# An attention head with a PSUM bank pair per item, and remainders and state additions ahead of the spline in every fourth step

## The reference

```python
f = 1.0 / (1.0 + np.exp(-f_logit))
for t in range(S):
    state = f[:, :, t, :, None] * state + np.einsum('bhd,bhe->bhde', k[:, :, t], v[:, :, t])
    y[:, :, t] = np.einsum('bhd,bhde->bhe', q[:, :, t], state)
# x = y as (3072, 384); layer 1, w_in 384 x 2048, w_out 2048 x 384:
h = x @ w_in
x = np.where(h >= 1, h, np.where(h <= -1, 0, (h + 1) ** 2 / 4)) @ w_out
# layer 2, same shapes:
h = x @ w_in2
P = a[0] + a[1] * h + a[2] * h**2 + a[3] * h**3
Q = 1.0 + abs(b[0]) * abs(h) + abs(b[1]) * h**2
out = (P / (Q + 1e-6)) @ w_out2
```

## Time and profile before

| | us |
|---|---|
| median of 3 runs | 1020.75 |
| lowest, highest | 1018.28, 1024.6 |
| the profiled execution's own time | 1022.0 |
| its span | 1020.3 |

### The profile page before, as it was taken

How to read it: one execution, slowest core, us unless ns; L and a number is a source line. 1 busy time by engine, 2 the same in 40 slices (tenths; PEclk the granted TensorE clock), 3 DMA queues, 4 the chain that set the end, 5 groups by cost and what they waited for, 6 DMA issues and landing times.

```text
span 1020.3 us, 12881 instructions
## 1 busy us (share of the span) xinstructions
PE 938.0 (92%) x4626; PEld 756.8 (74%) x4626; DVE 747.9 (73%) x909; ACT 573.0 (56%) x725; POOL 253.5 (25%) x138
## 2 busy tenths in 40 slices
PE   3589898988999899989989997999999999999996
PEld 3467777777777777777778775788888888888885
DVE  6677775666666666657735669998888888888884
ACT  4434433443433344334324468888878788787872
POOL 4123320000001000000003433523434435243223
PEclk9698889999999999999999998999999999999999
DMA  5333321211121121113012231001001010010000
GB/s 163 96 95 90 92 63 51 74 32 31 51 59 31 31 79 32 45 47 87 1 32 75 80 93 62 1 1 62 0 21 41 0 62 0 0 62 0 31 1 34
DMA packets 27510, 48.68 MB, mean 48 GB/s; under 512 B 5312, under 2 KB 8384, under 8 KB 27456
## 3 DMA queue, kind: packets, MB, share of 16 engines
q1 hardware_dynamic: 27456, 48.00, 15.9%
HBM read 36.18 MB, written 9.44 MB: 45 GB/s over the span
## 4 chain that ended last, share of the span: by engine, by line
PE 72%; DVE 15%; ACT 6%; issue 5%; POOL 1%; POOLq 0%; DMA 0%; SPq 0%; ACTq 0%; DVEq 0%
PE acc L1086 18%; PE h_pair L1026 14%; PE acc L1042 13%; PE at_pair L1064 9%; PE h_pair L1064 9%; DVE t L832 4%; PE at_pair L971 3%; DVE g L839 3%; DVE x_lo L827 2%; ACT t L589 2%; PE at_pair L989 2%; PE at_bank L998 1%; PE at_pair L984 1%; ACT g_hi L596 1%; DVE growth L765 1%
## 5 line engine op out<-in xcount | busy, mean ns | idle before, releaser
L832 DVE SCALAR_TENSOR_TENSOR t<-t 128x512 f32<-128x512 f32 x96 | 85.7, 893 | 127.7 <-ACT t L589 126.8
L487 POOL TENSOR_TENSOR g_lo<-g,g_hi 128x1024 fp32r<-128x1024 f32 x48 | 116.7, 2431 | 233.1 <-DVE t L867 228.6
L589 ACT ACTIVATE t<-h_pair,half 128x512 f32<-128x512 f32 x96 | 65.9, 687 | 162.2 <-PE h_pair L1026 161.2
L596 ACT CAST g_hi<-g 128x512 fp32r<-128x512 f32 x96 | 59.5, 620 | 148.9 <-DVE g L839 148.3
L1026 PE MATMUL h_pair<-x_hi,w_hi 128*128 128x512 f32 x288 | 116.8, 405 | 16.1 <-DVE x_lo L827 15.6
L1042 PE MATMUL acc<-g_hi,w_hi 128*128 128x512 f32 x288 | 119.6, 415 | 0.0
L449 POOL TENSOR_TENSOR k_s<-k_in,growth 128x512 f32<-128x512 f32 x24 | 32.9, 1371 | 342.0 <-DVE growth L765 342.0
L1042 PE MATMUL acc<-g_hi,w_lo 128*128 128x512 f32 x288 | 115.8, 402 | 0.0
L1042 PE MATMUL acc<-g_lo,w_hi 128*128 128x512 f32 x288 | 115.7, 402 | 0.0
L1086 PE MATMUL acc<-g_hi,w_hi 128*128 128x512 f32 x288 | 113.8, 395 | 1.5 <-POOL g_lo L487 1.4
L1026 PE MATMUL h_pair<-x_lo,w_hi 128*128 128x512 f32 x288 | 114.8, 399 | 0.0
(11 more groups left out here) (106 smaller groups left out, 2020.1 us busy)
## 6 DMA issues: line engine op xcount, KB each, us to landing
w_raw<-w SPq DMA_DIRECT2D x32, 384.0 KB, 3.3
f_in<-fC SPq DMA_DIRECT2D x48, 96.0 KB, 2.8
k_in<-kC SPq DMA_DIRECT2D x48, 96.0 KB, 2.4
q_in<-qC SPq DMA_DIRECT2D x48, 96.0 KB, 2.3
v_in<-vC SPq DMA_DIRECT2D x24, 192.0 KB, 2.6
mlp_out<-o_sb SPq DMA_DIRECT2D x18, 256.0 KB, 3.2
x_raw<-mlp_out SPq DMA_DIRECT2D x6, 768.0 KB, 4.4
outT<-o_sb SPq DMA_DIRECT2D x18, 256.0 KB, 2.0
```

Of the source, the lines that this page charges most:

```text
L487: nc.gpsimd.tensor_tensor(g2_lo[r][:, :, :], g2[r][:, :, :], g2_hi[r][:, :, :].bitcast(F32), ALU.subtract).then_inc(lo2_ready, 1)
L589: nc.scalar.activation(t1[n % 2][:, :], h1[n % 2], ACT.Relu, scale=0.5, bias=half[:, :]).then_inc(relu1_ready, 1)
L596: nc.scalar.copy(g1_hi[n % R1][:, :], g1[n % 2][:, :]).then_inc(hi1_ready, 1)
L832: nc.vector.scalar_tensor_tensor(out=t1[n % 2][:, :], in0=t1[n % 2][:, :], scalar=1.0, in1=t1[n % 2][:, :], op0=ALU.min, op1=ALU.mult).the ...
```

## The change

In the head each item has its own two PSUM banks, `score_ps[i]`: the first for its scores and outputs, the second for its scores of the other head, then for its transposes (which wait for `masked`) and deltas. Items 2 and 3 put their scaled keys into `o_sb[0]` and `o_sb[1]`. The sequences of the head are new on PE, ACT, POOL and DVE; SP's is as before. `deltas(2)` and `deltas(3)` come behind the first halves of steps 0 and 1, and the first half of step 1 waits for `states(1)`, since it writes item 1's second bank. In every fourth step (stage 3) `rest_y(i)` and `states(i)` come ahead of the square.

```diff
-        score_ps = [[at_pair[:, 0:NB], at_pair[:, NB:2 * NB]], h1]
-        misc_ps = [at_bank, *acc]
+        score_ps = [[at_pair[:, 0:NB], at_pair[:, NB:2 * NB]], h1, [acc[0][:, :], acc[1][:, :]], [at_bank[:, :], acc[2][:, :]]]
...
         def scores_at(i):
-            return (score_ps[i % 2], i - 2) if i < HEAD else (score_ps[0], i - 2 if i == HEAD else i - 1)
+            return (score_ps[i], -1) if i < HEAD else (score_ps[0], 0 if i == HEAD else i - 1)
         def misc_at(i):
-            return (misc_ps[i], -1) if i < HEAD else (misc_ps[0], 0 if i == HEAD else i - 1)
+            return score_ps[i][1] if i < HEAD else at_bank[:, :]
+        def k_scaled(i):
+            return o_sb[i - 2] if 2 <= i < HEAD else k_s[i % 2]
...
             def scale_keys(i):
...
-                if i >= 2:
-                    pool.wait_ge(scores_ready, i - 1)
-                    pool.wait_ge(kt_ready, min(i - 1, ITEMS - GROUPS))
+                before = i - HEAD if i < HEAD + 2 else i - 2
+                if before >= 0:
+                    pool.wait_ge(scores_ready, before + 1)
+                    pool.wait_ge(kt_ready, min(before + 1, ITEMS - GROUPS))
...
             scale_keys(1)
+            scale_keys(2)
+            scale_keys(3)
             split_w1(0)
-            scale_keys(2)
             split_w1(1)
-            scale_keys(3)
             split_w1(2)
...
             invert(1)
+            gate_steps(2)
+            gate_steps(3)
+            invert(2)
+            round_y(0)
             copy_keys(0)
+            round_y(1)
             split_w1(0)
-            gate_steps(2)
-            round_y(0)
+            invert(3)
             copy_keys(1)
+            round_y(2)
             split_w1(1)
-            invert(2)
-            gate_steps(3)
-            round_y(1)
+            split_w1(2)
+            gate_steps(4)
+            round_y(3)
             copy_keys(2)
-            invert(3)
-            round_y(2)
+            invert(4)
             copy_keys(3)
-            gate_steps(4)
-            split_w1(2)
-            round_y(3)
-            invert(4)
             gate_steps(5)
...
             def newton(i):
...
-                if i >= 2:
+                if i >= HEAD + 2:
                     dve.wait_ge(y_done, i - 1)
+                elif i >= 2:
+                    dve.wait_ge(scores_ready, i - 1)
...
             newton(1)
+            scale_queries(1)
             mask(0)
-            scale_queries(1)
             scan(2)
+            mask(1)
             rest_y(0)
-            mask(1)
             newton(2)
...
             scale_queries(3)
-            states(0)
             rest_y(2)
             mask(3)
+            states(0)
+            states(1)
             scan(4)
-            states(1)
             rest_y(3)
...
             for n in range(N1):
                 i, stage = window_of(n)
+                if stage == 3:
+                    rest_y(i)
+                    states(i)
                 spline_square(n)
                 spline_max(n)
...
-                if stage == 3:
-                    rest_y(i)
-                    states(i)
...
             def transposes(i):
...
-                if before >= 0:
-                    pe.wait_ge(delta_done, 2 * (before + 1))
+                if i < HEAD:
+                    pe.wait_ge(masked, 2 * (i + 1))
+                elif i > HEAD:
+                    pe.wait_ge(delta_done, 2 * i)
...
             def scores(i):
...
+                if i == HEAD:
+                    pe.wait_ge(delta_done, 2)
...
             def spline_first(n):
...
+                elif n == 1:
+                    pe.wait_ge(delta_done, 4)
...
             pe.wait_ge(shaped, 2)
-            first_half(0)
-            first_half(1)
-            second_half(0)
-            first_half(2)
-            second_half(1)
-            first_half(3)
-            second_half(2)
-            second_half(3)
+            scores(0)
+            scores(1)
+            outputs(0)
+            transposes(0)
+            outputs(1)
+            transposes(1)
+            scores(2)
+            deltas(0)
+            outputs(2)
+            transposes(2)
+            scores(3)
+            deltas(1)
+            outputs(3)
+            transposes(3)
             for n in range(N1):
                 i, stage = window_of(n)
                 spline_first(n)
+                if n < 2:
+                    deltas(n + 2)
```

More of the change, by code:

```diff
@@ L445, in scale_keys @@
                 pool.wait_ge(growth_ready, GROUPS * (i + 1))
-                if i >= 2:
-                    pool.wait_ge(scores_ready, i - 1)
-                    pool.wait_ge(kt_ready, min(i - 1, ITEMS - GROUPS))
-                nc.gpsimd.tensor_tensor(k_s[u][:, :], k_in[u][:, :], growth[u][:, :], ALU.mult).then_inc(k_ready, 1)
+                before = i - HEAD if i < HEAD + 2 else i - 2
+                if before >= 0:
+                    pool.wait_ge(scores_ready, before + 1)
+                    pool.wait_ge(kt_ready, min(before + 1, ITEMS - GROUPS))
+                nc.gpsimd.tensor_tensor(k_scaled(i)[:, :], k_in[u][:, :], growth[u][:, :], ALU.mult).then_inc(k_ready, 1)
             def split_w1(k):
@@ L552, in copy_keys @@
                 act.wait_ge(kt_ready, i + 1)
-                nc.scalar.copy(k_nat[:, :], misc_at(i)[0][:, :]).then_inc(knat_ready, 1)
+                nc.scalar.copy(k_nat[:, :], misc_at(i)).then_inc(knat_ready, 1)
             def round_y(i):
@@ L813, in states @@
                     at = slice(HS * h, HS * h + HS)
-                    term = misc_at(i)[0][at, 0:BATCH * 2 * DH].rearrange("p (b h e) -> p b h e", h=2, e=DH)[:, :, h, :]
+                    term = misc_at(i)[at, 0:BATCH * 2 * DH].rearrange("p (b h e) -> p b h e", h=2, e=DH)[:, :, h, :]
                     total = state[r][at, :, HS * h:HS * h + DH]
@@ L950, in transposes @@
                     return
-                bank, before = misc_at(i)
                 pe.wait_ge(k_ready, i + 1)
-                if before >= 0:
-                    pe.wait_ge(delta_done, 2 * (before + 1))
+                if i < HEAD:
+                    pe.wait_ge(masked, 2 * (i + 1))
+                elif i > HEAD:
+                    pe.wait_ge(delta_done, 2 * i)
                 for b in range(BATCH):
                     at = slice(b * CK, (b + 1) * CK)
-                    mm = nc.tensor.transpose(bank[:, at], k_s[i % 2][:, at], ident[:, :])
+                    mm = nc.tensor.transpose(misc_at(i)[:, at], k_scaled(i)[:, at], ident[:, :])
                 mm.then_inc(kt_ready, 1)
@@ L970, in scores @@
                         at = slice(HS * h, HS * h + DH)
-                        mm = nc.tensor.matmul(banks[h][:, cols], k_s[u][at, cols], q_s[u][at, cols], start=True, stop=True)
+                        mm = nc.tensor.matmul(banks[h][:, cols], k_scaled(i)[at, cols], q_s[u][at, cols], start=True, stop=True)
                 mm.then_inc(scores_ready, 1)
@@ L997, in deltas @@
                 for b in range(BATCH):
-                    mm = nc.tensor.matmul(misc_at(i)[0][:, b * 2 * DH:(b + 1) * 2 * DH], k_nat[:, b * CK:(b + 1) * CK],
+                    mm = nc.tensor.matmul(misc_at(i)[:, b * 2 * DH:(b + 1) * 2 * DH], k_nat[:, b * CK:(b + 1) * CK],
                                           v_in[i % 2][:, b, :, :], start=True, stop=True)
```

## The result

The changed kernel takes 982.6 us (median of 4 runs, 981.24 to 982.73), the kernel before 1022.67 in the runs beside them; ratio 0.9613, interval 0.9591 to 0.9635. The forecast was 984.0 in a range of 975 to 995. The profiled execution took 982.7 us, its span is 981.0, against 1022.0 and 1020.3. Lines of the changed kernel are named with their new numbers: L1036 is the first half (L1026 before), L1052 the second, L963 the transposes, L979 the scores, L821 `states`, L828 and L832 `rest_y`, L837 the square, L844 the maximum, L850 the remainder.

What follows compares the result with a forecast made beforehand. PE was taken to bound the kernel, busy 92% of the span, with DVE and ACT slower in items 4 to 7. Gains of 7.6 (head included) and 30.2 us, 37.8 off 1022.0, gave 984 us, range 975 to 995.

Steps and rivals of the forecast that it cites:

- Items 8 to 23: Windows of these items: PE's waits for `states`, `rest_y` and scores all vanish, 25.1 us; with half clock 30.2 us.
- the half clock of 5.1: Items 8 to 23: three stretches of PE at half clock after chunk-edge waits vanish, 1.7 us each, 5.1 us.
- the 2.31 us hole: DVE's idle time before step 3's square, item 13's window; `rest_y` and `states`, 2.2 us, fit in it.
- Items 4 to 7: Windows where DVE with ACT is the slower chain: step 16 starts at 151.5 instead of 159.09, 7.6 us, head included.
- The head: Before step 0: its first half starts at 44.4 instead of 51.13, 6.7 us early, but only 0.3 us lasts.
- rival A: The head's lead lasts: the first square starts at 52.4, 3.4 us more gain, 981 us; chance 0.11.
- a sign of being wrong: Any of: first square near 52 or after 58, new cause of PE's waits between 160 and 530, half clock there.
- My lay-out: Head's instructions laid end to end with old durations, PE at half clock: `deltas(1)` end at 35.8, v(3) lands near 39.7.
- POOL beside the moved pair: Items 4 to 7: `rest_y` and `states` keep 2.2 us beside POOL's weight splits; if slowed, some 2 us less gain.
- the row at 78.08 that the prediction reads: Kernel before, items 4 to 7: `states` at 78.08 took its usual 0.72 us, read as evidence about POOL's splits.
- Rival E: `rest_y` ahead of the spline blocks DVE, needing 9.5 us in each of 19 windows: about 1032 us; chance 0.02.
- 6 us of room: Items 8 to 23: the square's maximum has 6 us to spare before the first half two steps on needs it.

Runs made afterwards that it cites:

- the move alone: Kernel before, its head unchanged, with `rest_y` and `states` ahead of the square in stage 3: 983.43 us, ratio 0.9611.
- the six executions at 95.6 to 96.0: Changed kernel, its order of stage 3 with the old head, six, twelve or twenty-four idle DVE products, and early `deltas(2)` and `deltas(3)`: 975.01 to 1094.33 us.
- the head alone: Changed kernel with `rest_y` and `states` back behind the spline's remainder in stage 3, new head kept: 1017.17 us, ratio 0.9943.
- the two kernels that take it away: Changed kernel with `states(3)` behind the first square, 977.92 us; changed kernel with `deltas(2)` and `deltas(3)` ahead of step 0, 975.01 us.
- the six-products kernel: Changed kernel with six idle DVE products between `states` and the square in stage 3, items 8 to 19: 993.95 us, ratio 0.9741.
- the three doses: Changed kernel with six, twelve or twenty-four idle DVE products ahead of stage 3's square, items 8 to 19: 993.95, 1028.07 and 1094.33 us.
- four executions: Without `rest_y` and `states` moved in items 4 to 7: new head 1017.17 us, or 987.34 moved from item 8; old head 1022.67, or 986.27 moved from item 8.
- identical program: Same up to step 16: changed kernel with `rest_y` and `states` behind the remainder everywhere, 1017.17 us, or only for items 4 to 7, 987.34 us.
- the early deltas without the move: Changed kernel with `deltas(2)` and `deltas(3)` ahead of step 0, but `rest_y` and `states` back behind the remainder: 1017.34 us, ratio 0.9955.

## Why the prediction was right, step by step

- *Items 8 to 23: all 25.1 us of waits, and the half clock of 5.1.* Measured 31.1: 25.3 of idle time and 5.8 of busy time. The waits are gone, the clock is 1.00. The regular window takes 21.4 us (transposes at 217.41 and 238.79 in the chain) where I wrote 21.5. Shown by the move alone.
- *The move fills the 2.31 us hole and the square waits for ACT anyway.* Shown by the row at 278.14, whose wait is 0.22 us.
- *Items 4 to 7: 7.6 us by DVE's chain.* Step 16 came 8.0 us early, states of items 4, 5 and 6 ended at 75.3, 101.9 and 128.5 for my 76.0, 102.4 and 128.7. From the first square to step 16 it is 95.6 us for 103.0, 7.4 less, where the forecast had 7.3 without the head's 0.3. That these windows are DVE's and ACT's with the move is shown by the six executions at 95.6 to 96.0. Without it PE's clock decides as well, and had the kernel before run them as the head alone did (98.5), the gain there would have been 2.9. In measured time the move in items 4 to 7 adds 3 to 5.
- *The head: 6.7 us early at step 0, 0.3 us left at the square.* It was 7.4 us early (43.74) and 0.8 left; the cause, deltas(3) behind the first half of step 1 with `states(3)` ahead of the first square, is shown by the two kernels that take it away. The size is in part luck: 0.8 goes with half clock in step 0, and the six-products kernel, with the same head at full clock, has its first square at 52.33, 3.8 us early, near what I had called rival A and a sign of being wrong. My lay-out had PE at half clock all the way; its instructions ran at full speed from about 19 us, so deltas(1) ended at 31.1 instead of 35.8, and were slow again behind the wait for v(3). That load still decided: v(3) landed at 39.1 (39.7 forecast), after PE had stood 7.9 us for it.
- *POOL beside the moved pair.* The pair kept 1.40 and 0.73 us, but this tests nothing: in the changed kernel no split of weights ran beside them in the windows of items 4 to 7 (in item 5's from 97.45 to 99.28 and from 106.00 to 107.82, the pair from 99.75 to 101.90). Nor does the row at 78.08 that the prediction reads, which ended before the split at 78.83 began. Two other rows of the kernel before do: `states` at 105.55 and 132.74 took 0.73 and 0.74 us with splits from 105.46 to 107.27 and from 132.66 to 134.47. The square beside such a split took 1.82 to 1.86. For `rest_y` no row shows it.
- *Rival E, slower because `rest_y` blocks DVE.* Rightly small here, but its price was wrong. I gave the square 6 us of room, from one instruction's lateness, and left out that DVE has to catch up before the next window; by the three doses the room is 1.8 us per window, and 5.5 us of added work in 12 windows made the kernel slower than before (ratio 1.0056). The "about 1032" doesn't follow either: 35 us on top of 984 are 1019. The step that failed is "it would take 9.5 us in each": with 1.7 us until DVE is held, 1.8 of room and 1.8 of loss, 5.3 would do.
- *The head alone*, in the expectations: 0.8 us was a fifth of what came. By four executions the new head reached step 16 between 0.4 and 6.5 us before the old one (152.63 and 156.75 for 159.09 and 157.19), which one profile of each does not let me divide into the edit and the clock.

## What to carry to other kernels

Where an in-order engine has a hole ahead of one instruction and another engine waits for something queued behind it, what is queued behind can fill the hole for nothing; read the hole's length and the time at which its end would have been reached anyway, and compare with the work to be moved. Do not read an engine's room off its busy share: count the waits between its own instructions that can't be filled, or dose it with idle work. And before the head of a pipeline is shortened, look for what stands first in the queue of the engine that bounds the next stage; here one state addition behind two moved multiplications held 5 to 8 us. And where a clock that falls after waits is in play, profile an identical program a second time before a few microseconds are put down to an edit.

## What the runs showed of the hardware

TensorE's clock fell to half after waits of 2.8 us in some places and not in others of the same length (159.1 and 347 us in the kernel before have the wait and keep 2.4 GHz; near 253, 441 and 526 they don't), after a wait of 2.54 us but not after one of 2.55 at the same point of an identical program, and in one kernel near 203 and 227 us, where no wait is longer than 1.6 us. The changed kernel, whose waits there are all gone, has it nowhere from step 16 to step 80. Seven executions of the changed kernel's head differ likewise: after waits for v(3) of 5.4 and 5.7 us the first half of step 0 took 2.34 us, after 6.8 and 6.9 it took 3.9 to 4.0, after 7.6 to 7.9 it took 4.21. The clock made 2.7 of the 4.1 us by which identical programs differ at step 16, and two stretches that cost 1.7 us each are together about what the early deltas without the move lost behind step 16.
